# Fused attention and two MLP layers: the turn of row statistics placed between scores and sums, with other instruction orders on four engines

## The reference

```
q_bits = (q @ proj > 0); k_bits = (k @ proj > 0)        # 6 bits: a bucket per row
scores = where(q_bucket == k_bucket, q @ k.T / sqrt(64), -1e9)
scores = scores - max(scores, axis=-1)
attn   = exp(scores) / (sum(exp(scores)) + 1e-9)
x      = attn @ v                       # 2 batches x 8 heads, 768 rows, head size 64
h      = x @ w_in;  g = max(h,0) + alpha * min(h,0);  y = g @ w_out       # 1536 x 512, inner 2048
h2     = y @ w_in2; g2 = P(h2) / (Q(h2) + 1e-6);      out = g2 @ w_out2   # P cubic, Q quadratic in |h2|
```

## Time and profile before

| | |
|---|---|
| median of the runs | 807.16 us |
| the profiled execution, its span | 805.88 us, 804.0 us |
| TensorE busy | 781.2 us (97%), 3820 matmuls |
| weight loads (PEld) | 585.5 us (73%) |
| VectorE busy | 531.5 us (66%) |
| ScalarE busy | 360.4 us (45%) |
| GpSimd busy | 271.4 us (34%) |
| granted TensorE clock | 1.00 |
| transfers | 58.85 MB, 73 GB/s over the span |

### The profile page before, as it was taken

One profiled execution on the slowest core, in us unless ns is written; L12 is line 12 of the kernel. 1 busy time (PEld: TensorE's weight loads), 2 busy tenths in 40 slices (PEclk: granted clock), 3 DMA queues, 4 the chain that ended last, 5 costly groups with the idle time before them and its releaser, 6 DMA issues.

```text
span 804.0 us, 11707 instructions
## 1 busy us (share of the span) xinstructions
PE 781.2 (97%) x3820; PEld 585.5 (73%) x3820; DVE 531.5 (66%) x822; ACT 360.4 (45%) x588; POOL 271.4 (34%) x341
## 2 busy tenths in 40 slices
PE   8889999989999999999999999999999999999998
PEld 5455656556566678888888888887888888888886
DVE  6766777667673654435333543379888988888886
ACT  7345555545545311102101201057667666676673
POOL 7584635635553769400000077782000000000000
PEclk9999999999999999999999999999999999999999
DMA  4575665665744143100000033330000100001001
GB/s 126 142 207 135 171 171 142 186 149 147 194 120 110 55 138 117 53 1 0 1 1 14 0 85 100 92 94 12 0 1 1 53 0 1 1 14 39 1 1 52
DMA packets 34206, 58.85 MB, mean 73 GB/s; under 512 B 9900, under 2 KB 13780, under 8 KB 34164
## 3 DMA queue, kind: packets, MB, share of 16 engines
q1 hardware_dynamic: 33876, 58.26, 26.7%
q10 hardware_dynamic: 288, 0.04, 0.0%
HBM read 29.59 MB, written 3.24 MB: 41 GB/s over the span
## 4 chain that ended last, share of the span: by engine, by line
PE 82%; SPq 5%; DVE 5%; DMA 4%; issue 2%; POOL 1%; ACT 1%; DVEq 0%; ACTq 0%
PE acc L1335 31%; PE ps_h L1303 31%; PE ps_o L590 6%; PE ps_a L505 4%; PE ps_s L565 3%; PE ps_s L560 3%; DMA q<-stats 3%; PE ps_o L611 1%; PE ps_a L501 1%; SPq L140 1%; PE ps_o L599 1%; DVE row_max L1002 1%; SPq L400 1%; PE ps_s L618 1%; DMA stage<-in_w_in 0%
## 5 line engine op out<-in xcount | busy, mean ns | idle before, releaser
L1368 ACT ACTIVATE g_hi<-num 128x512 fp32r<-128x512 f32 x96 | 60.0, 625 | 207.6 <-PE acc L1335 203.3
L1438 DVE TENSOR_TENSOR g_lo<-num,g_hi 128x512 fp32r<-128x512 f32 x96 | 72.3, 753 | 79.0 <-ACT g_hi L1368 78.4
L720 ACT ACTIVATE p<-ps_s 128x768 f32<-128x768 f32 x96 | 77.6, 812 | 77.6 <-PE ps_s L565 77.4
L1002 DVE TENSOR_REDUCE row_max<-ps_a 128x1 f32<-128x384 f32 x180 | 91.9, 551 | 29.5 <-PE ps_a L505 26.5
L1303 PE MATMUL ps_h<-x_hi,w_late_in_hi 128*128 128x512 f32 x288 | 78.9, 395 | 0.2 <-POOL w_late_in_lo L1267 0.2
L1303 PE MATMUL ps_h<-x_hi,w_late_in_lo 128*128 128x512 f32 x288 | 78.8, 394 | 0.0
L1303 PE MATMUL ps_h<-x_lo,w_late_in_hi 128*128 128x512 f32 x288 | 78.8, 394 | 0.0
L590 PE MATMUL ps_o<-p,v_use 128*64 128x384 f32 x384 | 73.2, 500 | 0.0
L1446 DVE TENSOR_SCALAR num<-ps_h,alpha_sb 128x512 f32<-128x512 f32 x48 | 36.0, 750 | 55.4 <-PE ps_h L1303 52.6
L1376 ACT ACTIVATE den_q<-ps_h,abs_b 128x512 f32<-128x512 f32 x48 | 33.0, 688 | 83.8 <-PE ps_h L1303 77.6
L1035 DVE TENSOR_TENSOR p_sum<-p 128x768 f32<-128x768 f32 x48 | 55.8, 1164 | 15.9 <-PE ps_o L611 12.8
(11 more groups left out here) (166 smaller groups left out, 1535.6 us busy)
## 6 DMA issues: line engine op xcount, KB each, us to landing
stage<-in_w_in SPq DMA_DIRECT2D x26, 256.0 KB, 2.8
stage<-in_w_out SPq DMA_DIRECT2D x26, 256.0 KB, 2.7
raw<-in_qk SPq DMA_DIRECT2D x15, 384.0 KB, 3.7
q<-hi SPq DMA_DIRECT2D x30, 192.0 KB
k<-hi SPq DMA_DIRECT2D x30, 192.0 KB
v_raw<-in_v SPq DMA_DIRECT2D x16, 192.0 KB, 4.4
work<-rden_scratch SPq DMA_DIRECT2D x16, 192.0 KB, 3.4
out<-y SPq DMA_DIRECT2D x12, 256.0 KB, 2.5
```

The costliest lines, as they stand in the source:

```text
L720: nc.scalar.activation(halves(p[c][:]), ps_s[c % 2][:, :, 0:HALF], ACT.Exp, scale=float(D) ** -0.5).then_inc(s_exp, 1)
L1002: dve.tensor_reduce(row_max[slot][:, i, c:c + 1], ps_a[:, i, 0:HALF], AX.X, ALU.max).then_inc(s_a_free, 1)
L1368: nc.scalar.activation(g_hi[f % 2][:], num[f % 4][:], ACT.Copy).then_inc(s_ghi, 1)
L1438: dve.tensor_tensor(g_lo[f % 2][:], num[f % 4][:], g_hi[f % 2][:], ALU.subtract).then_inc(s_glo, 1)
```

## The change

In all heads but 0 and 1, the turn moves from behind the values of chunks 0 and 1 to behind the scores of chunk 3, with sums directly behind it and bits after that; the row-max chunks are shifted by one place. Head 1 gets its own order. SP no longer issues the high parts of qa and ka; ScalarE's queue does, behind its rounding (for head 2, ahead of the pairs, SP still does). SP stages early weights at other places. ScalarE takes stat_rows before the fourth exponential, split_qk one chunk later, and x_high ahead of the next head's first exponential. GpSimd takes normalise ahead of split_qk, and split_weights elsewhere.

```diff
--- before.py
+++ after.py
@@ -281,19 +281,19 @@
                             ([("a", 2, 1)], [("a", 2, 2)]),
                             ([("a", 2, 3)], [("a", 2, 4)])]
                 if second_head:
-                    return [([("a", 1, 5)], [("m", 1, 0)]),
-                            ([("bits", 3, 0)], []),
-                            ([("a", 2, 0)], [("a", 2, 2)]),
-                            ([("a", 2, 1)], []),
-                            ([("a", 2, 3)], [("a", 2, 5)]),
-                            ([("a", 2, 4)], [])]
+                    return [([("a", 1, 5)], [("a", 2, 0)]),
+                            ([("bits", 3, 0)], [("m", 1, 0)]),
+                            ([("a", 2, 1)], [("a", 2, 3)]),
+                            ([("a", 2, 2)], []),
+                            ([("a", 2, 4)], []),
+                            ([("a", 2, 5)], [])]
                 more, bits = left > 0, left > 1 or (left == 1 and u == 0)
-                return [([("a", 2, 0)] if more else [], [("m", 1, 0)]),
-                        ([("bits", 3, 0)] if bits else [], []),
-                        ([("a", 2, 1)] if more else [], [("a", 2, 3)] if more else []),
-                        ([("a", 2, 2)] if more else [], []),
-                        ([("a", 2, 4)] if more else [], [("a", 2, 5)] if more else []),
-                        ([], [])]
+                return [([("a", 2, 0)] if more else [], [("a", 2, 1)] if more else []),
+                        ([("m", 1, 0)] + ([("bits", 3, 0)] if bits else []), []),
+                        ([("a", 2, 2)] if more else [], [("a", 2, 3)] if more else []),
+                        ([], []),
+                        ([("a", 2, 4)] if more else [], []),
+                        ([("a", 2, 5)] if more else [], [])]
 
             def group_of(first_head):
 
@@ -452,26 +452,18 @@
                     for u in range(2):
                         h = 2 * j + u
                         first = isinstance(j, int) and j == 0
-                        if left == 1 and u == 0:
-                            stage_early(2)
                         if left > 1:
                             load_raw(u, j + 2)
                         if left:
                             load_v(u, j + 1)
-                        if first:
-                            stage_early(u)
-                        if not left and u == 0:
-                            stage_early(3)
-                        if first and u == 0:
-                            fill_stats(1 - u, j + u)
-                        if left > 1 or (left == 1 and u == 0):
-                            fill_a_hi(1 - u, h + 3)
                         if not (first and u == 0):
                             store_sums(sp, 1 - u, j - 1 + u, h - 1, den_row[1 - u][:])
-                        if (left or u == 0) and not (first and u == 0):
+                        if left or u == 0:
                             fill_stats(1 - u, j + u)
                         if left > 1 or (left == 1 and u == 0):
                             fill_a_pen(1 - u, h + 3)
+                        if left == 1:
+                            stage_early(2 + u)
                         if u == 0 and not first:
                             turn_sums(sp, j - 1)
                         if left:
@@ -480,6 +472,8 @@
                             store_rows(sp, j - 1)
                         if left:
                             fill_b_lo(u, j + 1)
+                        if first:
+                            stage_early(u)
                         if u == 0 and not first:
                             spread(sp, j - 1)
 
@@ -658,6 +652,7 @@
                         first = isinstance(j, int) and j + u == 0
                         steps = uses_of(left, u, first, isinstance(j, int) and j == 0 and u == 1)
                         group = group_of(first)
+                        due_sums = not first
                         for begin in range(0, KC, group):
                             for c in range(begin, begin + group):
                                 t = KC * h + c
@@ -670,13 +665,17 @@
                                     if kind == "m":
                                         turn(*at, n)
                                         b = 1 - b
+                                        if due_sums:
+                                            sums(h - 1)
+                                            due_sums = False
                                     else:
                                         use(kind, *at, cc, n, b)
                                     n = n + 2
                                 if final:
                                     early_up(pe, u, c)
-                            if begin == 0 and not first:
+                            if due_sums:
                                 sums(h - 1)
+                                due_sums = False
                             for c in range(begin, begin + group):
                                 values(u, h, c, KC * h + c)
                                 if c == 3:
@@ -703,6 +702,13 @@
                     if due(128 * jj):
                         act.wait_ge(s_b_in[u], 128 * jj)
                     nc.scalar.activation(hi[u][:], raw[u][:], ACT.Copy).then_inc(s_hi, 1)
+
+                def fill_a_hi(u, g):
+
+                    act.wait_ge(s_hi, g + 1)
+                    act.wait_ge(s_a_out, a_chunks_done(g - 2))
+                    act.dma_start(qa[u][0:D].bitcast(F32), hi[u][0:D].bitcast(F32)).then_inc(s_a_in[u], 16)
+                    act.dma_start(ka[u][0:D].bitcast(F32), hi[u][D:P].bitcast(F32)).then_inc(s_a_in[u], 16)
 
                 def copy_v(u, jj):
                     g = 2 * jj + u
@@ -809,20 +815,23 @@
                         last = final and u == 1
                         for c in range(KC):
                             t = KC * h + c
-                            if c == (3 if first and u == 0 else 2) and not last:
+                            if c == (3 if first and u == 0 else 1) and not (last or (first and u == 1)):
                                 stat_rows(1 - u, j + u)
+                            if c == 4 and u == 1 and not first:
+                                x_high(act, j - 1)
                             if c + 2 < KC:
                                 exponential(c + 2, h, t + 2)
                             elif not last:
                                 exponential(c + 2 - KC, h + 1, t + 2)
                             if c == 1 and not (first and u == 0):
                                 sums_of(1 - u, j - 1 + u, h - 1)
-                            if c == (4 if first and u == 0 else 1) and (left > 1 or (left == 1 and u == 0)):
+                            if c == 1 and first and u == 1:
+                                stat_rows(0, 1)
+                            if c == (4 if first and u == 0 else 2) and (left > 1 or (left == 1 and u == 0)):
                                 split_qk(1 - u, j + 1 + u)
+                                fill_a_hi(1 - u, h + 3)
                             if c == 3 and not last:
                                 copy_v(1 - u, j + u)
-                            if c == (2 if final else 5) and u == 1 and not first:
-                                x_high(act, j - 1)
                         if last:
 
                             act.wait_ge(s_xlo, PAIRS - 1)
@@ -956,25 +965,29 @@
 
                 def pair(j, left):
                     final = not left
+                    first = isinstance(j, int) and j == 0
                     for u in range(2):
                         h = 2 * j + u
                         if not (final and u == 1):
                             if not (isinstance(h, int) and h == 0):
                                 v_partial(1 - u, j + u)
                             row_stats(1 - u, h + 1)
+                        if first and u == 1:
+                            split_weights(0)
+                        if left == 1:
+                            split_weights(1 + u)
+                        if final and u == 0:
+                            split_weights(3)
                         if left > 1 or (left == 1 and u == 0):
                             bit_rows(1 - u, j + 1 + u)
-                            split_qk(1 - u, j + 1 + u)
-                        if left == 1 and u == 0:
-                            split_weights(2)
                         if u == 1 and not final and not (isinstance(j, int) and j == 0):
                             normalise(j - 1)
+                        if left > 1 or (left == 1 and u == 0):
+                            split_qk(1 - u, j + 1 + u)
+                        if u == 1 and not final and not (isinstance(j, int) and j == 0):
                             x_low(j - 1)
-                        if isinstance(j, int) and j == 0:
-                            split_weights(u)
                         if final and u == 0:
                             normalise(j - 1)
```

(1 more changed line is left out.)

## The result

The changed kernel takes **803.23 us** (median of nine; 801.71 to 804.27) against 807.16 (805.92 to 810.94). The ratio on record is 0.9926, interval 0.9899 to 0.9953; the two medians by themselves give 0.9951, the upper end of it, so the gain is 4 to 6 us. That is a real gain and a small one; the forecast of 795.0 missed it by 8 us, and the range ended 0.2 us under it. What follows explains those.

What follows compares the result with a forecast made beforehand. TensorE, busy for 97% of the span, was taken as the bound, with only its idle time in the attention to win. 16.3 us won less 4.0 lost, net 12.3, gave 794.9 from 807.16, called 795.0; range 789.8 to 803.

Steps and rivals of the forecast that it cites:

- (6): GpSimd series before the even heads' turn: new mcols stall of 0.1 to 1.5 us in five even heads, 2.5 lost.
- Rival A: GpSimd's series decides every even turn at its long end, 1.5 instead of 0.5: 5 us back, 800.0; chance 0.15.
- (7): Neighbours: GpSimd overlapping VectorE's add in odd heads, 1.0 us lost in five; later split_weights(0) in head 2, 0.5 lost.
- (4): Turn's waits for mcols: head 1 wins 1.2 us, head 14 wins 0.8, sum 2.0.
- (2): Statistics' transfer on SP leaves earlier: TensorE's waits shrink, 4.1 us won in the loop plus 2.0 in head 0, 6.1.
- Rival B: Statistics come no earlier because bytes, not issues, stood ahead: 6.1 us less, 801.1, or 799.1 if only the loop; chance 0.13.
- (1): Turn ahead of sums and values: v_sum waits go, 3.5 us in five odd heads and 1.1 in head 1, sum 4.6.
- (3): Row-max chunk order: less TensorE blocking on VectorE's row maxima, 0.28 us in each of 13 heads, 3.6 won.
- its sign: Weight loader's waits for row_max were to be about three per head less one.
- (5): Row-max operands issued on ScalarE's queue: 1.2 us per head, hidden by 1.4, so cost nothing.
- The final transition: End of the attention: x_low of pair 6 moves later by about one exponential, before work waiting for a weight load: 0.

## Why the prediction was wrong

**(6) GpSimd is the step that failed**, in size, not in mechanism. The place, the landing (13.46 after line 593; forecast 13.15 to 14.55) and the due time (118.53, that is 21.6; forecast 21.35) were right; the series was 9.43 instead of 8.3, so mcols came at 22.9, beyond the long end of 22.85. The waits of the five pairs were 1.40, 1.41, 1.58, 1.40 and 1.33, together 7.1 against 2.5: near the long end of the 0.1 to 1.5 that I had given, where the sum took 0.5. Rival A, with a chance of 0.15, is what happened, and in every pair. The missing 1.1 had been in my hands: (7) priced the overlap of adds and GpSimd on VectorE's side alone, 0.2 a head, and took GpSimd's instructions at their lengths from places where nothing ran beside them. The row that I used, an add of 2.46 beside normalise, says that one of the two is held; which one depends on who came first. In the changed kernel the add came first, it kept its 0.95, and GpSimd paid. The rule of the Trainium skill that I weighed and rated too low (GPSIMD Engine Reference, Key points: contention with VectorE's instructions of two SBUF inputs) holds here: v_three's spacing is 0.66 alone and 1.38 beside an add, normalise's 1.81 and 2.40. I had also reasoned that "most such adds have slack behind them", which is true of the adds and beside the point, because GpSimd had none.

**(4) mcols of head 14** had the wrong sign: forecast 0.8 won, measured 2.7 lost, as a wait of 2.18 instead of 1.02 and some 1.7 of slow clock. mcols did come earlier than before (22.7 instead of 24.1 after the even head's line), but the turn moved up by more, and the forecast never set the one against the other there as (6) does for the loop. Contention is the smaller part of it: v_three is long again (1.31), normalise (1.86) is not. The forecast said that no term comes from the clock, since it stood at 1.00 in the profile; a change that makes a longer wait can bring it in, and the runs with x_low twice, with x_high in its old place and with split_qk first show that it often does.

**(2)** was right in the loop: no statistics wait is left there (forecast 4.1 of 4.4). In head 0 it was 0.8, not 2.0 (wait 2.33 to 1.51): I had charged the wait to issues and bytes ahead of it, and the run with nothing ahead shows that the transfer's own 3.0 us hold it. Rival B, bytes ahead of it, is not the reason either.

**(1)** was right on v_sum: 4.8 us of waits to none. Head 1's turn kept a wait of 0.57, now for the row maxima, where I had 1.2 won for (4).

**(3)** came out in size: TensorE's busy time fell by 0.54 a pair, 0.27 a head against 0.28. Its mechanism isn't shown: the run with the last row-max chunk moved alone had 0.13 a pair, so most of the fall came with the other moves, and no run says which. What I had offered as its sign was wrong too: the weight loader's waits rose to 18.6 us in 51, while the busy time fell; that more of them now fall where a matmul is running anyway is argued, not shown.

**(5)** costs nothing on the path, as forecast: TensorE waits for ScalarE once, 0.8 us, as before. But "nothing" was written beside a gain that I had not priced: the queue is worth some 2 to 5 us, and without it no gain of the change is clear of noise (0.9993). My sum reached those microseconds through (1) and (2).

**(7), head 2**: 0.5 forecast, 0.4 lost. The final transition is right.

The sum, profile to profile: forecast 12.3; 4.6 less for the five even turns, 3.8 less for head 14, 2.2 less for heads 0 and 1, and 0.1 less in the rest: 1.6. The version with x_low moved, at 794.06, is about where the forecast was, in part by luck: its five pairs won 9.1 us (forecast 6.9), its heads 0 and 1 2.5 (forecast 4.3).

## What to carry to other kernels

When a change places a run of instructions of one engine on the path, price that run with its new neighbours, and price a contention on both sides: the engine without slack is the one that counts. If the margin between "ready" and "due" is smaller than the error of the series (here 0.1 to 1.5 us short, with an error of 1.1), forecast the stall, and look at once for the instruction in it that nobody needs soon; moving x_low by one head was worth more than twice the whole change. In an in-order queue a wait is paid by everything behind it: ask of each part of a reordering whether it works without the others.

## What was not expected of the hardware

TensorE's granted clock fell to 0.50 behind single waits in a kernel that is otherwise busy, and stayed there for some 3.4 us each time (6.8 once). In the changed kernel, behind the wait of 2.18 us that ended at 243.99:

```profile
244.00:245.30 1.30, 1.30 (x27) 1.05 (x27) 0.29 (x1) 0.72 (x3) 1.22 (x3) 1.00 0.00 0
245.40:248.70 3.30, 3.30 (x14) 1.28 (x11) 3.09 (x2) 0.68 (x2) 3.00 (x2) 0.50 0.02 5
```

It can be behind a wait of 1.39 us (x_high in its old place, 33.60) and not behind one of 3.13 (the same kernel, 91.34) or 3.11 (x_low twice, 226.93). Two windows behind waits for the statistics, of 1.73 us (105.91) and 1.75 us (139.32), in the kernel before with split_qk one exponential later:

```profile
106.00:108.00 2.00, 2.00 (x12) 1.57 (x14) 1.25 (x3) 1.12 (x2) 0.00 (x0) 1.00 0.21 29
...
139.00:142.00 3.00, 2.68 (x8) 2.42 (x8) 1.31 (x3) 0.81 (x1) 0.00 (x0) 0.54 0.22 34
```

The wait is the same and the clock is not (1.00 and 0.54). The length of the wait alone doesn't decide it, and what does was not tried. It makes the cost of a stall jump: 1.8 us more of GpSimd cost 2.9 to 3.1 a pair where the clock fell and 1.8 where it did not.

GpSimd's instructions are lengthened by nearly all the time for which they lie beside a two-input add: v_three started 0.16 into an add of 1.01, so 0.85 of the add lay beside it, and took 0.72 longer; normalise started 0.23 into one of 0.95, 0.72 beside it, and took 0.59 longer. Where GpSimd starts first, VectorE is the one that is held: its add of 0.96 took 2.46 when it began 0.22 into normalise.
